# Splitting the first quarter of the next expert weights in two pieces, the first of them between a ReLU and a copy

## The chip, the cores and the metric

The kernel runs on one core of a Trainium2 chip. The metric is the device time of one execution in microseconds (us); lower is better. The engines are named as in the profile: PE (TensorE matmuls), PEld (its weight loads), ACT (ScalarE), DVE (VectorE), POOL (GpSimd), SP (SyncE, which issues transfers).

## The reference

Three stages: a thresholded attention, a dense layer with squared ReLU, and eight experts, of which each token takes one. The change touches the third:

```python
# N, D, E, F = 2304, 512, 8, 1024
logits = x @ w_gate
e_idx = np.argmax(logits, axis=1)
...
for e in range(E):
    mask = e_idx == e
    ...
    h = np.maximum(x[mask] @ w1[e], 0.0)
    ye = h @ w2[e]
    out[mask] = gate_w[mask, None] * eom[mask, e, None] * ye
```

Everything is in float32.

## The kernel before

A matmul in full float32 precision is replaced by three in a faster format (fp32r): each operand is split into a high part (a copy rounded to fp32r) and a low part (the operand minus its high part), and high x high, high x low and low x high are summed. So every operand is written twice before PE reads it: the high part by ACT, the low part by DVE or POOL.

The expert stage sorts the tokens by expert into *slots* of 128 tokens, each with one expert. There are at least 18 and at most 25 slots; how many there are, and which expert each has, is known only on the chip. With these inputs there are 22 (88 high-part copies of weights, four a slot). A slot's steps:

- the 128 rows of x are gathered (POOL's indirect DMA), transposed on PE into `xt_ps` and split into `x_gT_hi` (ACT) and `x_gT_lo` (DVE);
- `hidden`: two groups g = 0, 1 of 12 matmuls each (128x512) fill `he_ps0` and `he_ps1`;
- ACT applies the ReLU (`relu`, into `h_sb`), PE transposes four blocks for each group into `ht_ps`, ACT (`split_h`, into `h_T_hi`) and DVE (`h_T_lo`) split them;
- `output`: again two groups of 12 matmuls, into `oe_ps`; DVE scales the sum into `o_sb` and POOL stores it by indirect DMA.

The transposes stand inside the products: those of the first half of h after two of the four chunks of `hidden`'s second group, those of the second half after the first chunk of `output`. The next slot's x is transposed between `hidden` and `output`.

The weights of one expert are 128 x 8192 float32 in a raw buffer, of which there are three (`w_experts`). There is only one pair of split buffers, `w_hi` and `w_lo`, each in four quarters of 128 x 2048: quarters 0 and 1 are w1 (the two groups of `hidden`), 2 and 3 are w2 (the two groups of `output`). In every slot all four quarters are split anew for the next slot, each as soon as PE has finished with it. A quarter is written once the group that reads it is complete: semaphores `he_done` and `y_done` count these groups. ACT counts its high parts in `hi_done`, DVE its low parts (quarters 0 to 2) in `lo_dve`, POOL its (quarter 3) in `lo_pool`, and PE waits for `lo_dve` or `lo_pool` before each group.

The order of the work is written out by hand, one instruction stream for each engine. ACT's of a slot t (`slot` in the scalar block): high part of quarter 3 (of slot t's own weights), ReLU of the first half, copy of the first half of h, ReLU of the second half, copy of the next x, copy of the second half of h, and high parts of quarters 0, 1 and 2 for slot t + 1. DVE's: low part of the first half of h, of the next x, of the second half of h, low parts of quarters 0 and 1, the scaling, low part of quarter 2. The first slots and the last of the 18 sure ones are written out, the ones between run in a hardware loop (of three slots a pass on PE and DVE, one on ACT), and the slots behind the 18th stand in nested conditions. SP loads expert e + 3 into its buffer when POOL and DVE have split the last slot that uses expert e.

Of the kernel before, what the change touches and what calls it, by code (L numbers as in the profile page):

```python
# [19 lines left out]
ALU = mybir.AluOpType  # L20
# [935 lines left out]

RING = 3
BUF, NEED = 0, SLOTS
ENDS = 2 * SLOTS


def experts(nc, w1, w2, y_rows, out, con):
# [4 lines left out]
    with ExitStack() as ctx:  # L967
# [131 lines left out]

        def split_lo(eng, alu, t, g, buf, done):  # L1100
            eng.wait_ge(hi_done, 4 * t + g + 1)
            alu.tensor_tensor(group_of(w_lo, g), raw_group(buf, g), group_of(w_hi, g).bitcast(F32),  # L1102
                              ALU.subtract).then_inc(done, 1)

        @block.sync
        def _(sp):
# [4 lines left out]
            def load(e):  # L1111
                n = (e % BUFS) * WE
                if e >= BUFS:

                    end = sp.value_load(control[0:1, ENDS + e - BUFS:ENDS + e - BUFS + 1], min_val=0, max_val=SLOTS)
                    wait_first(sp, lo_dve, 3 * end + 1, sp_on)
                    wait_first(sp, lo_pool, end + 1, sp_on)
                sp.dma_start(w_raw[:, n:n + KC * FE].rearrange("p (c f) -> p c f", c=KC),
                             w1[e].rearrange("(c p) f -> p c f", p=P)).then_inc(w1_in[e % BUFS], 16)
                sp.dma_start(w_raw[:, n + KC * FE:n + WE].rearrange("p (c f) -> p c f", c=FEC),  # L1120
                             w2[e].rearrange("(c p) f -> p c f", p=P)).then_inc(w2_in[e % BUFS], 16)
# [22 lines left out]
        def _(pool):  # L1144
# [16 lines left out]
            def split(t):  # L1161
                buf = weight_buffer(pool, t)
                split_lo(pool, nc.gpsimd, t, 3, buf, lo_pool)

# [42 lines left out]
        def _(pe):  # L1207
# [26 lines left out]
            def products(out, lhs_hi, lhs_lo, c0, g, ahead_of=None, between=None):  # L1234

                for c in range(4):
                    if c == ahead_of:
                        between()
                    w = [x[:, g, c * 512:(c + 1) * 512] for x in (w_hi, w_lo)]
                    for n, (lhs, rhs) in enumerate(((lhs_hi, w[0]), (lhs_hi, w[1]), (lhs_lo, w[0]))):  # L1240
                        last = pe.matmul(out, lhs[:, c0 + c, :], rhs, start=(g != 3 and c == 0 and n == 0),  # L1241
                                         stop=(g != 2 and c == 3 and n == 2))
                return last

            def hidden(t):
# [3 lines left out]
                for g in range(2):  # L1249
                    pe.wait_ge(lo_dve, 3 * t + g + 2)  # L1250


                    products(h_ps[g][:], x_hi, x_lo, 0, g, ahead_of=2 if g else None,
                             between=lambda: h_transposed(t, 0)).then_inc(he_done, 1)
# [9 lines left out]
            def output(t, p):  # L1264
                pe.wait_ge(scaled, t + 1)
                for g in range(2):
                    pe.wait_ge(hlo_done, 2 * t + g + 1)
                    if g == 0:
                        pe.wait_ge(lo_dve, 3 * t + 4)
                    else:  # L1270
                        pe.wait_ge(lo_pool, t + 2)

                    products(oe_ps[p][:], h_hi, h_lo, 4 * g, 2 + g, ahead_of=None if g else 1,
                             between=lambda: h_transposed(t, 1)).then_inc(y_done, 1)
# [18 lines left out]
        def _(act):  # L1293
# [26 lines left out]

            def split_w(t, g, weights):
                buf, need = weights
                if g % 2 == 0:
                    wait_first(act, w1_ready if g == 0 else w2_ready, need, act_on)
                if not static(t) or t >= 1:

                    act.wait_ge(he_done if g < 2 else y_done, 2 * t - 1 + g % 2)  # L1327
                nc.scalar.activation(group_of(w_hi, g), raw_group(buf, g), ACT.Copy).then_inc(hi_done, 1)  # L1328

            def slot(t, first, more):  # L1330
                if not first:
                    split_w(t, 3, (weight_buffer(act, t), None))
                if more:
                    following = weights_of(t + 1)
                relu(t, 0)
                split_h(t, 0)
                relu(t, 1)
# [3 lines left out]
                if more:  # L1341
                    split_w(t + 1, 0, following)
                    split_w(t + 1, 1, following)
                    split_w(t + 1, 2, following)

            act.wait_ge(control_done, 1)
            weights = weights_of(0)
            split_w(0, 0, weights)
            split_w(0, 1, weights)
            split_x(0)  # L1350
            split_w(0, 2, weights)
            split_w(0, 3, weights)
            slot(0, True, True)
# [5 lines left out]
        def _(dve):  # L1359
# [101 lines left out]
            def slot(t, p, more):  # L1461
# [4 lines left out]
                if more:  # L1466
                    buf = weight_buffer(dve, t + 1)
                    split_lo(dve, nc.vector, t + 1, 0, buf, lo_dve)
                    split_lo(dve, nc.vector, t + 1, 1, buf, lo_dve)
                scale(t, p)  # L1470
                if more:
                    split_lo(dve, nc.vector, t + 1, 2, buf, lo_dve)

            buf = weight_buffer(dve, 0)
            split_lo(dve, nc.vector, 0, 0, buf, lo_dve)
            split_lo(dve, nc.vector, 0, 1, buf, lo_dve)
            split_x(0)
            split_lo(dve, nc.vector, 0, 2, buf, lo_dve)
            for t in range(RING):
# [41 lines left out]
```

## Time and profile before

| | us |
|---|---|
| median of 3 runs | 1074.66 (1074.55 to 1075.87) |
| profiled execution, its own time | 1075.23 |
| span of the profiled execution | 1073.4 |
| first matmul of the expert products to the last slot's first | 780.87 to 1052.14 |
| a slot, in the loop | 12.73 to 12.76 |
| PE busy over the span | 1017.6 (95%) |

Times of rows are us from the start of the span. A row of a timeline has the start, the duration, the engine, the line of the kernel, the operation, and output<-inputs. In brackets stands the idle time of the engine before it and what ended it. A matmul's row is longer than the interval to the next one, since matmuls are pipelined: the interval between starts is the time that one costs. PEld rows are the weight loads that run one matmul ahead.

### The profile page before, as it was taken

Reading aid. Unit: us, or ns where it says so; the run is one execution under the profiler, and the core shown is the slowest. Engines: PE = TensorE matmul, PEld = TensorE weight load, DVE = VectorE, ACT = ScalarE, POOL = GpSimd, SP = SyncE. Lnnn points to the kernel's source line nnn. Section 1 sums busy time; section 2 is a strip of 40 time slices with the busy share of each in tenths; the row PEclk is TensorE's granted clock in tenths of the full one; section 3 lists DMA queues with packets and bytes.
Section 4 is the critical chain, followed back from the end, with each engine's and each line's share of the span. In section 5 each row is a group of like instructions: output and inputs, shape, how many; then the busy total and the mean of one; then the engine's idle time right before and its main releaser. Section 6 shows DMA issues by size and latency. Waiting matters only on the chain. (4 is left out here: it accounts for less than half of the span.)

```text
span 1073.4 us, 19432 instructions
## 1 busy us (share of the span) xinstructions
PE 1017.6 (95%) x6901; PEld 840.3 (78%) x6901; DVE 612.5 (57%) x1137; ACT 596.3 (56%) x902; POOL 461.1 (43%) x725
## 2 busy tenths in 40 slices
PE   7999999999998999999999999999299999999996
PEld 5778778778776888888888888899177777777774
DVE  5788788888784334222422422332757777777773
ACT  4777787777774334222322322233168888877773
POOL 4777777777772000000000000000347777777773
PEclk9999999999999999999999999999589999999999
DMA  4322322323112110000000000010981554510110
GB/s 111 83 51 69 82 51 77 74 63 77 39 28 71 49 40 1 20 20 1 10 20 10 0 20 20 1 31 11 349 326 39 198 209 172 193 39 32 40 39 33
DMA packets 78891, 75.16 MB, mean 70 GB/s; under 512 B 49103, under 2 KB 59855, under 8 KB 78802
## 3 DMA queue, kind: packets, MB, share of 16 engines
q1 hardware_dynamic: 75282, 63.49, 19.7%
q0 software_dynamic: 3520, 10.49, 3.0%
q8 instruction: 54, 0.88, 0.4%
q14 instruction: 35, 0.29, 0.1%
HBM read 64.52 MB, written 10.49 MB: 70 GB/s over the span
## 5 line engine op out<-in xcount | busy, mean ns | idle before, releaser
L915 DVE TENSOR_TENSOR g_buf<-r_buf 128x512 f32<-128x512 f32 (+1 forms) x80 | 51.1, 639 | 236.1 <-ACT r_buf L853 236.1
L1165 POOL MEMSET ones<- 128x128 bf16 x1 | 0.2, 210 | 416.0 <-POOLq L652 416.0
L853 ACT ACTIVATE r_buf<-h_ps 128x512 f32<-128x512 f32 (+1 forms) x80 | 44.4, 556 | 240.0 <-PE h_ps L799 240.0
L1328 ACT ACTIVATE w_hi<-w_experts 128x2048 fp32r x88 | 161.1, 1906 | 13.2 <-issue 13.2
L1102 POOL TENSOR_TENSOR w_lo<-w_experts,w_hi 128x2048 fp32r<-128x2048 f32 x22 | 138.8, 6307 | 64.5 <-ACT w_hi L1328 64.5
L1102 DVE TENSOR_TENSOR w_lo<-w_experts,w_hi 128x2048 fp32r<-128x2048 f32 x66 | 149.1, 2286 | 28.0 <-ACT w_hi L1328 28.0
L478 ACT ACTIVATE e_sb<-s_sb,stats,live 128x576 f32<-128x576 f32 x144 | 124.5, 865 | 22.4 <-POOL stats L264 21.0
L799 PE MATMUL h_ps<-x_hi,w_in_hi 128*128 128x512 f32 (+1 forms) x320 | 120.2, 376 | 2.3 <-DVE x_lo L901 2.3
L799 PE MATMUL h_ps<-x_hi,w_in_lo 128*128 128x512 f32 (+1 forms) x320 | 118.6, 371 | 0.0
L799 PE MATMUL h_ps<-x_lo,w_in_hi 128*128 128x512 f32 (+1 forms) x320 | 118.5, 370 | 0.0
L816 PE MATMUL y_ps<-g_hi,w_out_hi 128*128 128x512 f32 (+1 forms) x320 | 117.9, 368 | 0.0
L816 PE MATMUL y_ps<-g_lo,w_out_hi 128*128 128x512 f32 (+1 forms) x320 | 117.7, 368 | 0.0
L816 PE MATMUL y_ps<-g_hi,w_out_lo 128*128 128x512 f32 (+1 forms) x320 | 117.7, 368 | 0.0
L577 DVE SCALAR_TENSOR_TENSOR probs<-s_sb,stats,e_sb 128x576 f32<-128x576 f32 x144 | 115.3, 833 | 1.5 <-POOL stats L277 1.4
L568 DVE TENSOR_SCALAR_CACHE_REDUCE s_sb<-s_ps 128x576 f32<-128x576 f32 x144 | 103.8, 754 | 19.8 <-PE s_ps L354 18.6
L496 ACT ACTIVATE probs_T<-t_ps 128x384 f32<-128x384 f32 x192 | 86.7, 486 | 33.3 <-PE t_ps L369 28.2
L264 POOL TENSOR_SCALAR stats<-stats,minus_live 128x1 f32<-128x1 f32 x144 | 76.4, 531 | 61.3 <-DVE s_sb L568 60.7
L369 PE MATMUL t_ps<-ident,probs 128*128 128x128 f32 x576 | 87.9, 280 | 6.7 <-ACT probs_T L496 6.6
L369 PEld LDWEIGHTS t_ps<-ident,probs 128*128 128x128 f32 x576 | 64.9, 142 | 18.3 <-issue 17.9
L1241 PE MATMUL he_ps<-w_hi,x_gT_hi 128*128 128x512 f32 x176 | 74.0, 420 | 5.2 <-DVE w_lo L1102 2.1
L1241 PE MATMUL oe_ps<-w_hi,h_T_hi 128*128 128x512 f32 x176 | 72.9, 414 | 0.1
L799 PEld LDWEIGHTS h_ps<-x_hi,w_in_hi 128*128 128x128 f32 x320 | 60.8, 190 | 12.4 <-ACT x_hi L838 2.4
(190 smaller groups left out, 2228.3 us busy)
## 6 DMA issues: line engine op xcount, KB each, us to landing
w_experts<-in_moe_w_dram SPq DMA_DIRECT2D x16, 2048.0 KB, 9.6
y_rows<-y_row SPq DMA_DIRECT2D x36, 128.0 KB, 2.4
k_raw<-in_k_dram SPq DMA_DIRECT2D x32, 128.0 KB, 3.1
q_raw<-in_q_dram SPq DMA_DIRECT2D x32, 128.0 KB, 2.9
w_raw<-in_moe_w_in_dram SPq DMA_DIRECT2D x16, 256.0 KB, 3.1
v_nat<-in_v_dram SPq DMA_DIRECT2D x16, 256.0 KB, 2.6
y_T<-in_moe_w_out_dram SPq DMA_DIRECT2D x16, 256.0 KB, 2.6
v_odd<-in_v_dram SPq DMA_DIRECT2D x16, 64.0 KB, 2.3
```

Source lines behind the costliest of these rows:

```text
L264: V.tensor_scalar(stat(BIAS, step, h), stat(MAX, step, h), minus_live[:], None, ALU.mult).then_inc(bias_ready, 1)
L369: last = pe.transpose(out[:, j * P:(j + 1) * P], probs[c][:, blk * P:(blk + 1) * P], ident[:])
L478: nc.scalar.activation(e_sb[step % 2][h][:], s_sb[step % 2][h][:], ACT.Exp, bias=stat(BIAS, step, h), scale=live[:]).then_inc(exp_done, 1)
L496: nc.scalar.activation(out, src[:], ACT.Copy).then_inc(evac_done, 1)
L568: V.tensor_scalar(halves(s_sb[step % 2][h][:]), s_ps[n % 2][:, :, 0:HALF], 1.0, None, ALU.mult, ALU.max, accum_out=stat(MAX, step, h)).the ...
L577: V.scalar_tensor_tensor(probs_of(c, h), s_sb[step % 2][h][:], stat(CUT, step, h), e_sb[step % 2][h][:], ALU.is_ge, ALU.mult, accum_out=su ...
L799: last = pe.matmul(h_ps[:, f % 2, 0:cols], w, x[:, kc, 0:cols], start=(kc == 0 and m == 0), stop=(kc == KC - 1 and m == 2))
L816: last = pe.matmul(y_ps[d][:, 0:cols], w, g[f % 2][:, 0:cols], start=(f == 0 and m == 0), stop=(f == FC - 1 and m == 2))
L915: V.tensor_tensor(g_buf[:, 0:cols], r_buf[:, 0:cols], r_buf[:, 0:cols], ALU.mult).then_inc(sq_done, 1)
L1102: alu.tensor_tensor(group_of(w_lo, g), raw_group(buf, g), group_of(w_hi, g).bitcast(F32), ALU.subtract).then_inc(done, 1)
L1241: last = pe.matmul(out, lhs[:, c0 + c, :], rhs, start=(g != 3 and c == 0 and n == 0), stop=(g != 2 and c == 3 and n == 2))
L1328: nc.scalar.activation(group_of(w_hi, g), raw_group(buf, g), ACT.Copy).then_inc(hi_done, 1)
```

## The change

The high and low part of quarter 0 are each made in two pieces of 128 x 1024 (the chunks 0 and 1, and 2 and 3). The first high piece goes between the ReLU and the copy of the first half of h on ACT, the second stays behind the copy of the second half of h, ahead of quarter 1. DVE makes both low pieces where the low part of quarter 0 was. A list `PARTS` numbers the five pieces (quarter, first chunk, end chunk), and the counts that PE, SP and the engines wait for are changed to it (4 low parts of DVE in each slot where there were 3, 5 high parts where there were 4). PE's own order does not change: `ahead_of` counts matmuls now and no chunks, at the same places.

```diff
+PARTS = ((0, 0, 2), (0, 2, 4), (1, 0, 4), (2, 0, 4), (3, 0, 4))
+NPARTS = len(PARTS)
...
-        def split_lo(eng, alu, t, g, buf, done):
-            eng.wait_ge(hi_done, 4 * t + g + 1)
-            alu.tensor_tensor(group_of(w_lo, g), raw_group(buf, g), group_of(w_hi, g).bitcast(F32),
-                              ALU.subtract).then_inc(done, 1)
+        def split_lo(eng, alu, t, part, buf, done):
+            g, c0, c1 = PARTS[part]
+            eng.wait_ge(hi_done, NPARTS * t + part + 1)
+            alu.tensor_tensor(group_of(w_lo, g)[:, c0:c1], raw_group(buf, g)[:, c0:c1],
+                              group_of(w_hi, g)[:, c0:c1].bitcast(F32), ALU.subtract).then_inc(done, 1)
...
-                    wait_first(sp, lo_dve, 3 * end + 1, sp_on)
+                    wait_first(sp, lo_dve, (NPARTS - 1) * end + 1, sp_on)
...
                 for c in range(4):
-                    if c == ahead_of:
-                        between()
                     w = [x[:, g, c * 512:(c + 1) * 512] for x in (w_hi, w_lo)]
                     for n, (lhs, rhs) in enumerate(((lhs_hi, w[0]), (lhs_hi, w[1]), (lhs_lo, w[0]))):
+                        if 3 * c + n == ahead_of:
+                            between()
...
                 for g in range(2):
-                    pe.wait_ge(lo_dve, 3 * t + g + 2)
-
-
-                    products(h_ps[g][:], x_hi, x_lo, 0, g, ahead_of=2 if g else None,
+                    pe.wait_ge(lo_dve, (NPARTS - 1) * t + g + 3)
+
+
+                    products(h_ps[g][:], x_hi, x_lo, 0, g, ahead_of=6 if g else None,
...
-            def split_w(t, g, weights):
+            def split_w(t, part, weights):
                 buf, need = weights
-                if g % 2 == 0:
+                g, c0, c1 = PARTS[part]
+                if c0 == 0 and g % 2 == 0:
                     wait_first(act, w1_ready if g == 0 else w2_ready, need, act_on)
                 if not static(t) or t >= 1:
 
                     act.wait_ge(he_done if g < 2 else y_done, 2 * t - 1 + g % 2)
-                nc.scalar.activation(group_of(w_hi, g), raw_group(buf, g), ACT.Copy).then_inc(hi_done, 1)
+                nc.scalar.activation(group_of(w_hi, g)[:, c0:c1], raw_group(buf, g)[:, c0:c1], ACT.Copy).then_inc(hi_done, 1)
 
             def slot(t, first, more):
                 if not first:
-                    split_w(t, 3, (weight_buffer(act, t), None))
+                    split_w(t, 4, (weight_buffer(act, t), None))
                 if more:
                     following = weights_of(t + 1)
                 relu(t, 0)
+                if more:
+                    split_w(t + 1, 0, following)
                 split_h(t, 0)
                 relu(t, 1)
                 if more:
                     split_x(t + 1)
                 split_h(t, 1)
                 if more:
-                    split_w(t + 1, 0, following)
                     split_w(t + 1, 1, following)
                     split_w(t + 1, 2, following)
+                    split_w(t + 1, 3, following)
...
                     split_lo(dve, nc.vector, t + 1, 0, buf, lo_dve)
                     split_lo(dve, nc.vector, t + 1, 1, buf, lo_dve)
+                    split_lo(dve, nc.vector, t + 1, 2, buf, lo_dve)
                 scale(t, p)
                 if more:
-                    split_lo(dve, nc.vector, t + 1, 2, buf, lo_dve)
+                    split_lo(dve, nc.vector, t + 1, 3, buf, lo_dve)
```

What ACT issues in one pass of its loop, from the first ReLU on, before the change (`h_sb` is the ReLU, `h_T_hi` the copy of h, ISA and REGISTER_ALU are address and counter instructions):

```order
L1309 ACTIVATE h_sb<-he_ps0 128x512 [waits ht_set]
L1315 ACTIVATE h_T_hi<-ht_ps0 128x512 [waits y_done,ht_set]
L1306 REGISTER_ALU
L1309 ACTIVATE h_sb<-he_ps1 128x512 [waits ht_set,he_done]
L1300 REGISTER_ALU
L1302 REGISTER_ALU [waits xt_set]
L1303 ACTIVATE x_gT_hi<-xt_ps 128x512 [waits he_done]
L1315 ACTIVATE h_T_hi<-ht_ps1 128x512 [waits y_done,ht_set]
L1327 REGISTER_ALU [waits w1_ready]
L1328 ISA [waits he_done]
L1328 ACTIVATE w_hi<-w_experts 128x2048
```

And in the changed kernel, where ACT's lines are 4 or 5 higher:

```order
L1313 ACTIVATE h_sb<-he_ps0 128x512 [waits ht_set]
L1332 ISA [waits w1_ready]
L1333 ISA [waits he_done]
L1333 ACTIVATE w_hi<-w_experts 128x1024
L1319 ACTIVATE h_T_hi<-ht_ps0 128x512 [waits y_done,ht_set]
L1310 REGISTER_ALU
L1313 ACTIVATE h_sb<-he_ps1 128x512 [waits ht_set,he_done]
L1304 REGISTER_ALU
L1307 ACTIVATE x_gT_hi<-xt_ps 128x512 [waits he_done,xt_set]
L1319 ACTIVATE h_T_hi<-ht_ps1 128x512 [waits y_done,ht_set]
L1333 ISA [waits he_done]
L1333 ACTIVATE w_hi<-w_experts 128x1024
```

One 128x1024 piece moved ahead of the copy of the first half of h, with its wait for the weights (`w1_ready`); the other stands where the whole quarter stood.

What DVE issues in one slot of its loop, before, from the low part of the second half of h on:

```order
L1447 TENSOR_TENSOR h_T_lo<-ht_ps1,h_T_hi 128x512 [waits h_T_hi_done]
L1074 TENSOR_LOAD control
L1074 ISA x2
L1102 ISA [waits hi_done]
L1102 TENSOR_TENSOR w_lo<-w_experts,w_hi 128x2048
L1102 ISA [waits hi_done]
L1102 TENSOR_TENSOR w_lo<-w_experts,w_hi 128x2048
L1458 TENSOR_SCALAR o_sb1<-oe_ps1,place_factor 128x512 [waits y_done]
L1102 ISA [waits hi_done]
L1102 TENSOR_TENSOR w_lo<-w_experts,w_hi 128x2048
```

And now:

```order
L1454 TENSOR_TENSOR h_T_lo<-ht_ps1,h_T_hi 128x512 [waits h_T_hi_done]
L1077 TENSOR_LOAD control
L1077 ISA x2
L1106 ISA [waits hi_done]
L1106 TENSOR_TENSOR w_lo<-w_experts,w_hi 128x1024
L1106 ISA [waits hi_done]
L1106 TENSOR_TENSOR w_lo<-w_experts,w_hi 128x1024
L1106 ISA [waits hi_done]
L1106 TENSOR_TENSOR w_lo<-w_experts,w_hi 128x2048
L1465 TENSOR_SCALAR o_sb1<-oe_ps1,place_factor 128x512 [waits y_done]
L1106 ISA [waits hi_done]
L1106 TENSOR_TENSOR w_lo<-w_experts,w_hi 128x2048
```

The first 128x2048 subtraction became two of 128x1024, one behind the other; nothing else moved on DVE.

## Rows read from the trace of the kernel before

**Rows 1.** The page: busy us, share of the span and instructions of each engine.

```profile
PE 1017.6 (95%) x6901; PEld 840.3 (78%) x6901; DVE 612.5 (57%) x1137; ACT 596.3 (56%) x902; POOL 461.1 (43%) x725
```

**Rows 2.** Windows: us; PE, PEld, DVE, ACT, POOL busy (instructions); clock, DMA, GB/s.

```profile
859.77:974.50 114.73, 113.77 (x540) 91.14 (x541) 84.86 (x64) 91.14 (x82) 90.16 (x28) 1.00 0.41 144
```

**Rows 3.** The chain of waits, in order of time: start us, us, what.

```profile
870.15 2.30 DVE w_lo L1102
...
974.50 4.38 PE he_ps L1241 x18
...
987.33 4.37 PE he_ps L1241 x18
...
1038.48 4.37 PE he_ps L1241 x18
```

**Rows 4.** Timeline at a slot boundary: start, us, engine, instruction [idle before <-releaser].

```profile
871.29 0.39 PE L1241 MATMUL oe_ps<-w_hi,h_T_lo 128*128 128x512 f32 x1
...
871.97 0.39 PE L1241 MATMUL oe_ps<-w_hi,h_T_lo 128*128 128x512 f32 x1
872.50 0.19 PEld L1241 LDWEIGHTS he_ps<-w_hi,x_gT_hi 128*128 128x128 f32 x1 [0.56 <-DVE w_lo L1102]
...
872.84 0.40 PE L1241 MATMUL he_ps<-w_lo,x_gT_hi 128*128 128x512 f32 x1
```

**Rows 5.** Waits of the weight loads, 790 to 1053: us, times, longest.

```profile
PEld he_ps L1241 <- DVE w_lo L1102: 8.0, 15, 0.6
PEld he_ps L1241 <- issue: 4.5, 6, 1.5
```

**Rows 6.** Timeline at a slot boundary behind the loop.

```profile
1012.32 0.39 PE L1241 MATMUL oe_ps<-w_hi,h_T_lo 128*128 128x512 f32 x1
...
1013.25 0.40 PE L1241 MATMUL he_ps<-w_lo,x_gT_hi 128*128 128x512 f32 x1
```

**Rows 7.** Timeline at the start of the last slot.

```profile
1052.11 0.19 PEld L1241 LDWEIGHTS he_ps<-w_hi,x_gT_hi 128*128 128x128 f32 x1 [1.45 <-issue]
```

**Rows 8.** Timeline of ACT through one slot.

```profile
862.89 0.60 ACT L1309 ACTIVATE h_sb<-he_ps 128x512 f32<-128x512 f32 x1 [0.21 <-PE he_ps L1241]
864.62 0.60 ACT L1315 ACTIVATE h_T_hi<-ht_ps 128x512 fp32r<-128x512 f32 x1 [1.12 <-PE ht_ps L1261]
866.02 0.60 ACT L1309 ACTIVATE h_sb<-he_ps 128x512 f32<-128x512 f32 x1 [0.80 <-PE he_ps L1241]
866.54 0.60 ACT L1303 ACTIVATE x_gT_hi<-xt_ps 128x512 fp32r<-128x512 f32 x1
...
868.10 7.31 ACT L1328 ACTIVATE w_hi<-w_experts 128x2048 fp32r x4
```

**Rows 9.** Timeline of PE at the start of the output product.

```profile
865.83 0.60 PE L1231 MATMUL xt_ps<-ident,x_g 128*128 128x128 f32 x4
...
866.18 0.19 PEld L1241 LDWEIGHTS oe_ps<-w_hi,h_T_hi 128*128 128x128 f32 x1
```

**Rows 10.** Timeline of DVE through the same slot.

```profile
865.25 0.69 DVE L1447 TENSOR_TENSOR h_T_lo<-ht_ps,h_T_hi 128x512 fp32r<-128x512 f32 x1 [0.48 <-ACT h_T_hi L1315]
...
868.24 0.69 DVE L1447 TENSOR_TENSOR h_T_lo<-ht_ps,h_T_hi 128x512 fp32r<-128x512 f32 x1 [0.38 <-ACT h_T_hi L1315]
870.15 4.49 DVE L1102 TENSOR_TENSOR w_lo<-w_experts,w_hi 128x2048 fp32r<-128x2048 f32 x2 [1.22 <-ACT w_hi L1328]
...
875.23 2.28 DVE L1102 TENSOR_TENSOR w_lo<-w_experts,w_hi 128x2048 fp32r<-128x2048 f32 x1
877.98 0.69 DVE L1447 TENSOR_TENSOR h_T_lo<-ht_ps,h_T_hi 128x512 fp32r<-128x512 f32 x1 [0.48 <-ACT h_T_hi L1315]
```

**Rows 11.** Timeline of POOL in the same slot.

```profile
862.89 6.38 POOL L1102 TENSOR_TENSOR w_lo<-w_experts,w_hi 128x2048 fp32r<-128x2048 f32 x1 [2.28 <-ACT w_hi L1328]
```

**Rows 12.** Weight load at the second half of the output product.

```profile
869.32 0.19 PEld L1241 LDWEIGHTS oe_ps<-w_hi,h_T_hi 128*128 128x128 f32 x1
```

**Rows 13.** The page: transfers of expert weights, KB each, us to landing.

```profile
w_experts<-in_moe_w_dram SPq DMA_DIRECT2D x16, 2048.0 KB, 9.6
```

More of the change, by code:

```diff
@@ L1162, in split @@
                 buf = weight_buffer(pool, t)
-                split_lo(pool, nc.gpsimd, t, 3, buf, lo_pool)
+                split_lo(pool, nc.gpsimd, t, NPARTS - 1, buf, lo_pool)
             nc.gpsimd.memset(ones[:], 1.0).then_inc(pool_set, 1)
@@ L1268, in output @@
                     if g == 0:
-                        pe.wait_ge(lo_dve, 3 * t + 4)
+                        pe.wait_ge(lo_dve, (NPARTS - 1) * (t + 1) + 1)
                     else:
                         pe.wait_ge(lo_pool, t + 2)
-                    products(oe_ps[p][:], h_hi, h_lo, 4 * g, 2 + g, ahead_of=None if g else 1,
+                    products(oe_ps[p][:], h_hi, h_lo, 4 * g, 2 + g, ahead_of=None if g else 3,
                              between=lambda: h_transposed(t, 1)).then_inc(y_done, 1)
@@ L1341, in slot @@
                 if more:
-                    split_w(t + 1, 0, following)
                     split_w(t + 1, 1, following)
                     split_w(t + 1, 2, following)
+                    split_w(t + 1, 3, following)
             act.wait_ge(control_done, 1)
             weights = weights_of(0)
-            split_w(0, 0, weights)
-            split_w(0, 1, weights)
+            for part in range(3):
+                split_w(0, part, weights)
             split_x(0)
-            split_w(0, 2, weights)
-            split_w(0, 3, weights)
+            for part in range(3, NPARTS):
+                split_w(0, part, weights)
             slot(0, True, True)
@@ L1469, in slot @@
                     split_lo(dve, nc.vector, t + 1, 1, buf, lo_dve)
+                    split_lo(dve, nc.vector, t + 1, 2, buf, lo_dve)
                 scale(t, p)
                 if more:
-                    split_lo(dve, nc.vector, t + 1, 2, buf, lo_dve)
+                    split_lo(dve, nc.vector, t + 1, 3, buf, lo_dve)
             buf = weight_buffer(dve, 0)
-            split_lo(dve, nc.vector, 0, 0, buf, lo_dve)
-            split_lo(dve, nc.vector, 0, 1, buf, lo_dve)
+            for part in range(3):
+                split_lo(dve, nc.vector, 0, part, buf, lo_dve)
             split_x(0)
-            split_lo(dve, nc.vector, 0, 2, buf, lo_dve)
+            split_lo(dve, nc.vector, 0, 3, buf, lo_dve)
             for t in range(RING):
```

## Prediction

> **What bounds the kernel now.** I read the page first. PE is busy for 95% of the span and the other engines for less than 60% [rows 1]; in nine slots of the expert stage it is busy 113.77 of 114.73 us, at a granted clock of 1.00, which is its 2.4 GHz level [rows 2]. So only what PE itself loses can be won, and it is small. Where it loses anything is told by the chain of waits [rows 3]: in each slot it leaves PE once, for a high part on ACT and a low part of 2.30 us on DVE that starts at 870.15 and ends at 872.45. This is the low part of quarter 0, which the first matmul of the next slot needs.
>
> The timeline shows the price. Near the end of a slot matmuls start every 0.227 us (871.29 to 871.97 is three of them) [rows 4]. Then the load of the next slot's first weights, which would have started with the matmul at 871.97, starts only at 872.50, 0.05 after the low part ended, and the second matmul of the slot starts at 872.84. From 871.97 to there are 0.87 us where two undisturbed intervals take 0.454: PE loses 0.42 us. It is two things, the wait (0.30) and a restart in which the first load is not hidden (0.11).
>
> The waits of the loads count such boundaries [rows 5]: 15 ended by DVE's low part, 8.0 us, and 6 ended by "issue", 4.5 us, of which the longest is 1.5. The 15 are those of the loop; they idle 0.533 us on average against 0.56 in the one I measured, so on average they lose 0.42 - 0.03 = 0.39 us. The other six lie behind the loop. Five of them are alike: from 1012.32 to 1013.25 are 0.93 us, so 0.93 - 0.454 = 0.48 lost, and (4.5 - 1.45) / 5 = 0.61 idle on average against about 0.62 here gives 0.465 each [rows 5, 6]. I read them as the same wait for DVE, with one more instruction of PE's queue behind it. The sixth, before the last slot, is 1.45 us long [rows 7] and starts 0.9 us after DVE is through; I read it as PE's branch to another place of the program, which no low part shortens.
>
> **The change, part by part.**
>
> *First high piece, now behind the first ReLU.* ACT idles 1.12 us between the ReLU at 862.89 and the copy of h at 864.62 [rows 8], because PE must transpose in between. The piece is let go by what releases the ReLU itself, the end of the first group of `hidden`. A back-to-back successor of a 128x512 operation starts 0.52 later (866.02 to 866.54), and one of 128x2048 occupies (7.31 - 1.91) / 3 = 1.80 [rows 8]. No row has 128x1024; its bounds are these two, and on the line between them it occupies 0.52 + 1.28 / 3 = 0.95, which I take. It then starts at 862.89 + 0.52 = 863.41 and frees ACT at 864.36, 0.26 before the copy of h can start. Cost nothing, and the cover is 0.26 us thick. At the lower bound the spare is 0.69; at the upper one the copy would be 0.59 late. What is queued behind it is just that copy, and this matters: DVE's low part of h ends at 865.25 + 0.69 = 865.94 [rows 10], PE's load for the output product follows at 866.18, 0.35 behind the start of the transposes of x [rows 9]. I cannot tell from the rows which of the two sets it, so I count no spare behind the copy of h: every 0.1 us of delay there is 0.1 us of PE.
>
> The Trainium skill, "VectorE: DVE Perf Modes", section "The TRN2 errata", speaks against just this edit: an operation that reads SBUF pays a fixed cost, exposed between instructions, so many small tiles pay it each. By its ScalarE formula, 224 cycles plus one for each element at 1.2 GHz, the piece would take 1.04 us, as an estimate, all of it after the ReLU's end at 863.49, and end at 864.53: the spare would shrink to 0.09 and the sum stay as it is. This case's rows show operations starting 0.08 us before their predecessor ends (866.54 against 866.62), so the measurement is milder than the page.
>
> *ACT after the second copy of h.* The four copies run from 868.10 to 875.41 [rows 8]. Now it is half a quarter and three: quarter 1 is done at 868.10 + 0.95 + 1.91 = 870.96, quarter 2 starts at 870.85, quarter 3 at 872.65 and ends at 874.56, 0.85 earlier than now. Quarter 3 must not start before the last matmul of the slot is through at 871.97 + 0.39 = 872.36 [rows 4]; it does not. ACT's total rises by the fixed part of one operation, 0.1 us, on an engine with time to spare.
>
> *DVE.* It is free at 868.24 + 0.69 = 868.93 and today idles until 870.15 for the high part [rows 10]. Both high pieces are done before (the second at about 869.15), so the first low piece can start once its address is read; between 868.93 and 870.15 I take 869.2. A subtraction of 2048 takes 2.28 and occupies 4.49 - 2.28 = 2.21; one of 512 takes 0.69 [rows 10]. These are the bounds for 1024; on the line it takes 1.22 and occupies 1.15. The second piece ends at 869.2 + 1.15 + 1.22 = 871.57, 0.88 earlier than 872.45 and 0.35 before 871.92, from which a load at 871.97 would be late. So the wait goes wholly, restart included. At the upper bound the pieces would end at 873.7 and make every slot longer; each would have to occupy over 1.3 before anything of the gain is lost, which neither neighbour suggests. Quarter 1's low part then ends at 873.8, the scaling at 874.5 and quarter 2's low part at 876.7, ahead of the next low part of h, today at 877.98 and 0.4 earlier then.
>
> *What is late next.* POOL's low part of quarter 3 runs 862.89 to 869.27 [rows 11], and PE's load that needs it starts at 869.32 [rows 12], 0.05 behind its end: this pair is at its edge today. A faster slot alone would run into it. But POOL starts 0.2 after ACT's quarter 3, which comes 0.85 earlier, while PE comes 0.4 earlier: POOL gains 0.45 us of spare. The Trainium skill, "GPSIMD Engine Reference", section "Key points", says that POOL shares its SBUF interfaces with DVE and contends with instructions of two SBUF inputs, which these subtractions are. The rows do not show it: a slot of (974.50 - 872.50) / 8 = 12.75 us later [rows 3, 4] POOL runs again, from 875.64 on, DVE's subtraction at 875.23 runs to 877.51 beside it and takes 2.28, and the two at 870.15, with no subtraction on POOL, take 4.49 together [rows 10, 11].
>
> *Weights.* ACT waits for the next expert's weights 4.7 us earlier (863.4 for 868.1). The transfers land in 9.6 us (median) [rows 13] and start when a buffer comes free, two experts, so at least two slots or 25 us, ahead of their use. Nothing.
>
> *Sum.* 15 x 0.39 = 5.85, and 5 x 0.465 = 2.3: 8.15 us. In the first slot PE waits for the gathered x, in the last for its branch: no change. The profiled execution took 1075.23, so 1067.1 as the profile would have it. The median of the runs is 0.57 lower than this execution; from it 1066.5, which I forecast. About 0.2% (2.1 us) is what a measurement of this kernel can tell from no change.
>
> **Rivals.**
>
> *A, the copy of h becomes late (slower).* If the piece occupies ACT as a whole quarter does, 1.80, it frees ACT at 865.21, the copy of h is 0.59 late in 20 slots, and PE stops before the output product, again with a restart of 0.1. The slot wins 0.41 and loses 0.69: 20 x 0.28 = 5.6 slower, 1080. It decides from an occupation of about 0.95 + 0.26 + 0.3 = 1.5. Against it: durations grow evenly with the elements in the two rows I have. For it: no row has this shape, and a wait for weights and an address instruction stand between ReLU and piece.
>
> *B, half of it.* The piece goes, but 0.1 to 0.25 us of delay reach PE in each slot, by the queue instructions ahead of the copy of h or by a fixed cost on either engine. 20 x 0.15 to 20 x 0.25 less: 3 to 5 us of gain, 1070 to 1071.5. For it is the missing spare behind the copy of h.
>
> *C, no change.* Something else is due at the same moment as the low part: the next x, or PE's branches at the loop's end and in the conditions, of which rows 7 show that one can cost 1.45. If DVE's address read keeps the first piece near its old start, 870.15, the second ends at 870.15 + 1.15 + 1.22 = 872.5, as now: 1074.7. Against it: DVE has idled long before 870.15 and its release there is the high part.
>
> *D, the five boundaries behind the loop are bound by PE's own issue*, as the row's label says, and give nothing: 15 x 0.39 = 5.85, so 1068.8.
>
> **How the numbers follow.** Full gain 0.6 (1065.5 to 1067.7), D 0.1, B 0.12, C 0.1, A 0.08. The likeliest is 1066.5. A range of 1065.0 to 1071.5 leaves out C and A, and takes in the full gain, D and most of B. Faster by over 0.2%: 0.6 + 0.1 + 0.12 less a little for the thin end of B, 0.8. Within 0.2%: 0.12. Slower: 0.08.
>
> **What would show it.** Right: the 15 waits of loads for DVE's low part are gone, the first load of a slot starts 0.227 after its neighbour, slots in the loop last 12.35; ACT's 128x1024 rows take about 1.03 and the copy of h still starts 0.1 or less behind PE's transposes; DVE's are about 1.22. Wrong: an idle of PEld before the output product, ended by DVE's low part of h (A, B), or one at the slot's start that ends with "issue" (C, D), or POOL's low part named as the one waited for.

## The result and the profile after

| | before | changed |
|---|---|---|
| median, same chip (6 runs each) | 1075.2 us | 1065.77 us |
| profiled execution, its own time | 1075.23 us | 1065.43 us |
| its span | 1073.4 us | 1063.7 us |
| a slot in the loop, mean of 15 (before / here) | 12.75 us | 12.32 us |
| a slot behind the loop, mean of 4 | 12.79 us | 12.28 us |

The ratio is 0.9912, with an interval of 0.9899 to 0.9925: 0.9% faster. The forecast was 1066.5 with a range of 1065.0 to 1071.5.

First the boundary between two slots in the timeline of the changed kernel, which answers to [rows 4]:

```profile
867.99 0.39 PE L1245 MATMUL oe_ps<-w_lo,h_T_hi 128*128 128x512 f32 x1
...
868.22 0.39 PE L1245 MATMUL oe_ps<-w_hi,h_T_lo 128*128 128x512 f32 x1
868.22 0.19 PEld L1245 LDWEIGHTS he_ps<-w_hi,x_gT_hi 128*128 128x128 f32 x1
868.44 0.39 PE L1245 MATMUL he_ps<-w_hi,x_gT_hi 128*128 128x512 f32 x1
...
868.67 0.39 PE L1245 MATMUL he_ps<-w_lo,x_gT_hi 128*128 128x512 f32 x1
```

The next slot's first load starts with the last matmul of the slot and has no bracket any more, which means that it does not wait; from 868.22 to 868.67 there are two plain intervals, where [rows 4] have 0.87 us. All waits of weight loads from 780 to 1053 us, answering to [rows 5]:

```profile
PEld he_ps L1245 <- DVE x_gT_lo L1459: 1.8, 1, 1.8
PEld he_ps L1245 <- issue: 1.5, 1, 1.5
PEld oe_ps L1245 <- issue: 0.5, 1, 0.5
```

The 15 waits for DVE's low part and five of the six "issue" waits are gone. What is left is the first slot's wait for its x and the one before the last slot; the 0.5 for `oe_ps` lies inside the last slot, which [rows 5] did not reach. The windows of nine loop slots and nearly five behind them show PE busy without a gap (busy us of PE first, then its loads, DVE, ACT and POOL, then the clock):

```profile
856.12:967.02 110.90, 110.90 (x541) 91.89 (x540) 85.48 (x73) 91.71 (x91) 75.65 (x27) 1.00 0.42 150
979.34:1040.00 60.66, 60.66 (x298) 50.35 (x297) 46.75 (x41) 50.21 (x51) 39.92 (x15) 1.00 0.12 40
```

Nine slots took 114.73 us before [rows 2] and take 110.90. The timeline of ACT through the slot from 856.12 on, answering to [rows 8]:

```profile
859.11 0.60 ACT L1313 ACTIVATE h_sb<-he_ps 128x512 f32<-128x512 f32 x1 [0.64 <-PE he_ps L1245]
859.61 1.05 ACT L1333 ACTIVATE w_hi<-w_experts 128x1024 fp32r x1
860.84 0.60 ACT L1319 ACTIVATE h_T_hi<-ht_ps 128x512 fp32r<-128x512 f32 x1 [0.18 <-PE ht_ps L1265]
...
864.32 6.47 ACT L1333 ACTIVATE w_hi<-w_experts 128x1024 fp32r x4
```

The last row holds the second piece and quarters 1 to 3 back to back: 6.47 us where the four whole quarters took 7.31, so quarter 3 is done 0.84 earlier (the prediction has 0.85). The first piece, 1.05 us long, fills the idle time between ReLU and copy and leaves 0.18 of it; the copy of h is still let go by PE's transposes, 1.73 us behind the ReLU's start as before (862.89 to 864.62 in [rows 8]). DVE in the same slot, answering to [rows 10]:

```profile
864.46 0.69 DVE L1454 TENSOR_TENSOR h_T_lo<-ht_ps,h_T_hi 128x512 fp32r<-128x512 f32 x1 [0.41 <-ACT h_T_hi L1319]
865.42 4.56 DVE L1106 TENSOR_TENSOR w_lo<-w_experts,w_hi 128x1024 fp32r<-128x1024 f32 x3 [0.27 <-ACT w_hi L1333]
```

The row of 4.56 us holds both low pieces and quarter 1's low part. It starts 0.27 after the low part of h, where DVE idled 1.22 before; each piece takes 1.22 (mean of 44). POOL, answering to [rows 11], and PE's load for the second output group, to [rows 12]:

```profile
858.68 6.30 POOL L1106 TENSOR_TENSOR w_lo<-w_experts,w_hi 128x2048 fp32r<-128x2048 f32 x1 [3.47 <-ACT w_hi L1333]
...
866.42 1.11 POOL L1161 DMA_INDIRECT out_dram<-o_sb,place_token  x1 [0.30 <-issue]
```

```profile
865.49 0.19 PEld L1245 LDWEIGHTS oe_ps<-w_hi,h_T_hi 128*128 128x128 f32 x1
```

POOL ends at 864.98, 0.51 ahead of the load that needs it; before it was 0.05. Its store took 1.11 us where it took about 2.6; I come back to that. Last, the idle time before the last slot, to [rows 7], and the same row of a second profile of the changed kernel:

```profile
1041.98 0.19 PEld L1245 LDWEIGHTS he_ps<-w_hi,x_gT_hi 128*128 128x128 f32 x1 [1.49 <-issue]
```

```profile
1041.19 0.19 PEld L1245 LDWEIGHTS he_ps<-w_hi,x_gT_hi 128*128 128x128 f32 x1 [0.84 <-issue]
```

The same program idles there 0.8 us in one execution and 1.5 in another. A compare-and-branch of PE's queue (0.08 us) ends 0.13 us before the load at 1041.98, so the branch does stand in this gap; what fills the 1.3 us ahead of it no row shows.

**Where 9.7 us of span went.** Slots 2 to 16 take 6.46 us less together (184.81 for 191.27), and slots 17 to 21 take 2.14 less (62.67 for 64.81). The boundary behind the first slot gave 0.4. These 9.0 us are the change. The other 0.7 are not: the first slot started 0.68 earlier after a program that is the same up to there, PE's granted clock rose from 0.5 (its 1.2 GHz level) to 1.0 after 9 matmuls of the first slot in place of 12 (0.45 us), and the end behind the last slot's start took 0.4 longer. In two more profiles of the changed kernel the first slot lasted 14.31 and 14.52 us (14.34 here), the end 21.3 both times (21.7 here), and a loop slot 12.31 and 12.32.

### The profile page after: what moved, and what is told of

It reads as the page before. It is cut to its first block and busy times, and to the rows that moved or that the text cites. A ratio compares the mean times of both kernels' runs of the same rounds, so it can differ in the third digit from the quotient of the medians.

```text
span 1063.7 us, 19532 instructions
## 1 busy us (share of the span) xinstructions
PE 1008.9 (95%) x6901; PEld 839.9 (79%) x6901; DVE 613.9 (58%) x1159; ACT 597.8 (56%) x924; POOL 428.6 (40%) x725
## 5 line engine op out<-in xcount | busy, mean ns | idle before, releaser
L1333 ACT ACTIVATE w_hi<-w_experts 128x2048 fp32r (+1 forms) x110 | 165.4, 1565 | 14.2 <-issue 14.2
L1106 POOL TENSOR_TENSOR w_lo<-w_experts,w_hi 128x2048 fp32r<-128x2048 f32 x22 | 134.8, 6128 | 86.4 <-ACT w_hi L1333 86.4
L1106 DVE TENSOR_TENSOR w_lo<-w_experts,w_hi 128x1024 fp32r<-128x1024 f32 (+1 forms) x88 | 150.6, 1753 | 5.9 <-ACT w_hi L1333 5.3
L1245 PE MATMUL he_ps<-w_hi,x_gT_hi 128*128 128x512 f32 x176 | 71.6, 407 | 2.5 <-DVE x_gT_lo L1459 1.4
L799 PEld LDWEIGHTS h_ps<-x_hi,w_in_hi 128*128 128x128 f32 x320 | 60.3, 189 | 12.3 <-ACT x_hi L838 2.4
```

The source lines that it names most:

```text
L799: last = pe.matmul(h_ps[:, f % 2, 0:cols], w, x[:, kc, 0:cols], start=(kc == 0 and m == 0), stop=(kc == KC - 1 and m == 2))
L1106: alu.tensor_tensor(group_of(w_lo, g)[:, c0:c1], raw_group(buf, g)[:, c0:c1], group_of(w_hi, g)[:, c0:c1].bitcast(F32), ALU.subtract).then ...
L1333: nc.scalar.activation(group_of(w_hi, g)[:, c0:c1], raw_group(buf, g)[:, c0:c1], ACT.Copy).then_inc(hi_done, 1)
```

## Experiments

My theory: the quarter's low part no longer arrives late because DVE need not wait for a whole high part; taking half of that high part out of ACT's row behind the second copy of h also brings quarter 3, and so POOL, forward in step with PE; and the piece just fits before a copy of h that has no time to give. Rivals: splitting alone, or moving alone, is enough, or the pieces on DVE matter. The move and the split are taken out one at a time below. All results together, slots as means over the profile, ratios against the kernel before on the same chip:

| kernel | median us | ratio, interval | loop slot | behind the loop |
|---|---|---|---|---|
| split, nothing moved | 1067.61 | 0.9930, 0.9914 to 0.9947 | 12.41 | 12.37 |
| the same, POOL half | 1065.30 | 0.9911, 0.9896 to 0.9926 | 12.32 | 12.28 |
| whole quarter moved | 1075.96 | 1.0011, 1.0002 to 1.0021 | 12.88 | 12.66 |
| low part whole | 1065.08 | 0.9908, 0.9892 to 0.9925 | 12.32 | 12.29 |
| pieces 3 and 1 | 1067.14 | 0.9928, 0.9912 to 0.9945 | 12.45 | 12.29 |
| pieces 1 and 3 | 1064.97 | 0.9908, 0.9893 to 0.9923 | 12.32 | 12.28 |
| changed, again | 1065.15 | 0.9915, 0.9901 to 0.9928 | 12.31 | 12.28 |
| changed, third time | 1065.00 | 0.9909, 0.9894 to 0.9924 | 12.32 | 12.28 |

**Split, nothing moved.**

```diff
                 relu(t, 0)
-                if more:
-                    split_w(t + 1, 0, following)
                 split_h(t, 0)
...
                 if more:
+                    split_w(t + 1, 0, following)
                     split_w(t + 1, 1, following)
```

> Quarter 0 is split in two pieces as in the changed kernel, but the first high piece stays behind the copy of the second half of h; nothing is moved ahead. My theory: the first piece would be ready at once for DVE, whose two low pieces end as early as in the changed kernel, so PE no longer waits for them. But ACT reaches quarter 3 0.9 us later, so POOL's low part of quarter 3 (6.3 us) ends about 22.2 us after the start of the slot before, where PE's load wants it at 21.7. Half of that difference stays in every slot, with a restart: slots in the loop of about 12.6 us, the load of the output product's second half ended by POOL's low part in the list of waits, and 1072 us in all, 2 to 4 us under the kernel before. Rival 1, splitting alone is enough: slots of 12.33 and about 1066. Rival 2, the early piece is needed for the low part of quarter 0: slots of 12.75, the load at the slot's start ended by DVE's low part, 1075.

Its median is 7.3 us under the kernel before, where the changed kernel's is 9.4 to 9.7 under it: more than I expected, and yet not all. The loop slot is 12.41 where I had said 12.6. No load waits for the low part of quarter 0, so rival 2 is out. Waits of loads in this kernel, without the two that every kernel has:

```profile
PEld oe_ps L1245 <- issue: 1.6, 6, 0.5
...
PEld oe_ps L1245 <- POOL w_lo L1106: 1.4, 8, 0.2
PEld xt_ps L1235 <- DMA x_g<-y_rows,place_token: 1.2, 2, 0.9
```

POOL's low part is late, as the theory says, by up to 0.2 and not by 0.5 (the waits that end with "issue" are the same load in the slots behind the loop, and one in the last slot). I had reckoned with 6.3 us for it; here it takes 5.97, and I had charged a restart that a load 0.2 late hardly costs. A gather of x that comes late is a second wait that I did not foresee, and it is half of the loss: over the 15 loop slots this kernel loses 1.29 us against the changed one, 0.65 of them in the one slot that waits 0.9 for its gather. The gather in question takes 1.91 us of POOL's time where the changed kernel's take 0.99, and the last section tells why:

```profile
842.98 1.91 POOL L1154 DMA_INDIRECT x_g<-y_rows,place_token  x1
```

**The same with half of POOL's work.**

```diff
+                if t == 0:
+                    split_lo(pool, nc.gpsimd, t, NPARTS - 1, buf, lo_pool)
+                    return
+                pool.wait_ge(hi_done, NPARTS * t + NPARTS)
+                nc.gpsimd.tensor_tensor(group_of(w_lo, 3)[:, 0:2], raw_group(buf, 3)[:, 0:2],
+                                        group_of(w_hi, 3)[:, 0:2].bitcast(F32), ALU.subtract).then_inc(lo_pool, 1)
```

> As the kernel with the split alone (nothing moved ahead), but from the second slot on POOL subtracts only half of quarter 3 (128x1024), and the other half of that low part keeps the values of the first slot. If POOL's low part is what holds the kernel with the split alone back, it is now 3 us early and slots in the loop last 12.33 us, about 1066 in all, as in the changed kernel. If that kernel is held back by the low part of quarter 0 or by ACT, nothing changes against it.

12.32 us and no wait left in the slots. This kernel leaves out half of a low part, and with it both the late subtraction and the late gather go, since POOL issues the gather behind the subtraction. So with the split alone POOL is the bound, by both, and the split alone frees PE of the low part of quarter 0. What the move adds is time for POOL (0.09 us a slot).

**The whole quarter moved, no split.** `PARTS` has its four quarters, one high and one low operation for each, and the waits count them.

> Quarter 0 is not split; its whole high part (128x2048) stands between the first ReLU and the copy of the first half of h. The low part of quarter 0 and POOL's are then as early as in the changed kernel, so the waits at the slot's start go. My theory says that there is no spare behind the copy of h: the high part frees ACT 0.58 us after the copy could start, so the output product starts 0.55 to 0.6 late with a restart of 0.1, slots in the loop of about 13.0 us, with a wait of PE's load of the output product for DVE's low part of h, 1079 to 1081 us in all. Rival, half a us of delay is hidden behind the transposes and matmuls of PE: slots of 12.33 to 12.5, about 1066 to 1069, and the split was not needed at all.

No gain at all: 1.0 us slower than before by the medians, at the edge of what these runs can tell, and under the 1079 to 1081 that I expected. PE and ACT around the output product's start:

```profile
863.95 1.91 ACT L1333 ACTIVATE w_hi<-w_experts 128x2048 fp32r x1
...
865.75 0.59 ACT L1319 ACTIVATE h_T_hi<-ht_ps 128x512 fp32r<-128x512 f32 x1
...
866.38 0.60 PE L1235 MATMUL xt_ps<-ident,x_g 128*128 128x128 f32 x4
...
867.30 0.19 PEld L1245 LDWEIGHTS oe_ps<-w_hi,h_T_hi 128*128 128x128 f32 x1 [0.56 <-issue]
```

The copy of h has no bracket: it follows the high part at once, 2.30 us behind the ReLU's start in place of 1.73. The load for the output product is 0.56 late. The slot loses 0.57 against the copy and lasts 0.55 longer than in the changed kernel, so nothing behind the copy absorbs anything, but the restart of 0.1 that I charged is not there. Behind the loop the slot is only 0.37 longer: there is a spare of 0.2 there which I had not seen. It has two parts. This load starts 0.23 us behind the end of DVE's low part of h in the loop and 0.07 behind it in the later slots, and ACT's first ReLU starts 3.00 us into a slot in the loop and 2.92 in most of the later ones.

**Pieces of three chunks and one.**

```diff
-PARTS = ((0, 0, 2), (0, 2, 4), (1, 0, 4), (2, 0, 4), (3, 0, 4))
+PARTS = ((0, 0, 3), (0, 3, 4), (1, 0, 4), (2, 0, 4), (3, 0, 4))
```

> As the changed kernel, with quarter 0 split in pieces of 128x1536 and 128x512 in place of two of 128x1024, so the piece ahead of the copy of h is longer. On the line through the rows it occupies ACT for 1.37 us and frees it 0.15 us after the copy of h could start. My theory (no spare behind that copy): slots in the loop of 12.45 to 12.6 us, 1068.5 to 1071 in all, and a start of the copy that follows the end of the piece and no longer PE's transposes. Rival, some tenths of spare: slots of 12.33 and 1066.

The timeline of ACT:

```profile
860.29 0.60 ACT L1313 ACTIVATE h_sb<-he_ps 128x512 f32<-128x512 f32 x1 [0.77 <-PE he_ps L1245]
860.78 1.48 ACT L1333 ACTIVATE w_hi<-w_experts 128x1536 fp32r x1
862.16 0.59 ACT L1319 ACTIVATE h_T_hi<-ht_ps 128x512 fp32r<-128x512 f32 x1
```

The copy starts 1.87 behind the ReLU's start, 0.14 late, and a loop slot is 0.13 longer. Behind the loop nothing is lost, by the spare just named. So 1067.1, under my range of 1068.5 to 1071, which took all slots alike and a restart.

**Pieces of one chunk and three.** The same edit with `(0, 0, 1), (0, 1, 4)`.

> As the changed kernel, with pieces of 128x512 and 128x1536. The early piece is shorter, so ACT comes to quarter 3 about 0.43 us later than in the changed kernel, and POOL's low part ends just when PE's load wants it (spare of 0.45 less 0.43). My theory: slots of 12.33 to 12.38, 1066 to 1067. If POOL had more spare than I count, 12.33 exactly; if the early piece matters by more than POOL (the low part of quarter 0 ends later), over 12.4. The early piece occupies ACT for 0.52 us.

The loop slot of 12.32 is at the lower end of what I expected, the whole 1.0 us under my 1066 to 1067. I had left POOL nothing to spare; it ended 0.4 us ahead of its load (860.55 + 5.96 = 866.51 for 866.91), since its subtraction took 5.96 and not 6.3.

**Low part whole.**

```diff
             g, c0, c1 = PARTS[part]
+            c0 = 0
...
-                    split_lo(dve, nc.vector, t + 1, 0, buf, lo_dve)
                     split_lo(dve, nc.vector, t + 1, 1, buf, lo_dve)
```

The counts for `lo_dve` are those of three low parts a slot again.

> As the changed kernel on ACT, but DVE makes the low part of quarter 0 in one operation of 128x2048, once both high pieces are there. My theory: the second high piece is ready when DVE comes to it anyway, so the one operation ends at the time of the two, which PE does not wait for: slots of 12.33 and the time of the changed kernel within 0.1%, about 1066. Rival, the two low pieces bring part of the gain: slots of 12.4 to 12.75. On the side: POOL's indirect store took 2.64 us in the kernel before and 1.11 in the changed one. If it waits for the end of the DVE subtraction that runs when it starts (in the kernel before 1.74 us to that end plus 0.9; in the changed one 0.22 plus 0.9), it takes about 2.2 us here; if it depends on something else, it stays near 1.1 or returns to 2.6.

With the first high piece moved ahead, the two pieces on DVE bring nothing: one operation does as well, because the second high piece is done by 865.37 (864.32 + 1.05), 0.2 after DVE comes free. Without the move both high pieces would end at about 866.3 in the changed kernel's times, and one whole subtraction at about 868.7, 0.4 behind the load at 868.22: an estimate from these rows. A kernel with the high part split, the low part whole and nothing moved was not run. The side question is answered too, in the last section.

**The changed kernel again.**

> The changed kernel once more, for a second profile and a comparison on one chip with the other runs. Between the two profiles in hand the spans differ by 9.7 us; I account 9.0 of it to slot boundaries (8.6 to 9.0 by theory again here) and the rest to execution-to-execution differences before the first slot (0.7) and to when the clock rises in the first slot (0.4), against a tail 0.4 longer. If that is so, the start of the first slot and the moment of the clock's rise move between profiles of one kernel, and the slots in the loop stay at 12.33.

> The changed kernel, for a comparison on the same chip with the three orders of transposes: 12.33 us a slot in the loop, 1065 to 1066 in all. Only the time before the first slot, the clock's rise in it and the branch before the last slot should differ from the profiles in hand.

Both as expected; the numbers stand above.

**A better version?** What PE still loses is the restart behind its three groups of transposes. I put two groups together:

```diff
+            def h_then_x(t, p, more):
+                h_transposed(t, 0)
+                if more:
+                    x_transposed(t + 1, (p + 1) % RING)
...
-                    products(h_ps[g][:], x_hi, x_lo, 0, g, ahead_of=6 if g else None,
-                             between=lambda: h_transposed(t, 0)).then_inc(he_done, 1)
+                    products(h_ps[g][:], x_hi, x_lo, 0, g, ahead_of=5 if g else None,
+                             between=lambda: h_then_x(t, p, more)).then_inc(he_done, 1)
```

> The changed kernel with another order on PE: the transposes of the next x stand directly behind those of the first half of h, and both one matmul earlier. In the changed kernel PE stops nowhere at slot boundaries; each of the three groups of transposes costs 0.36 us and a longer first matmul behind it (0.32 where 0.227 is usual), so putting two together can save 0.09 us for each slot. But the output product starts 0.24 us behind the low part of h, which is PE's own delay from release to load, so it can only start earlier if the transposes of h do. They may be 0.1 us earlier before they meet the end of the ReLU. Theory: slots of 12.23 to 12.3, 0.5 to 2 us less than the changed kernel. Rival: the ReLU's end holds the transposes and nothing is won or 0.1 us for each slot is lost.

1070.36 us (0.9956, 0.9942 to 0.9969), loop slots of 12.50 where I had hoped for 12.23 to 12.3, slower than the changed kernel. The transposes of x had stood between the second ReLU and the transposes of its result; without them these came too early:

```profile
PEld ht_ps L1270 <- ACT h_sb L1315: 9.0, 21, 0.4
```

Three more, with `output`'s transposes moved as well (the first number is the place in `hidden`, the second the one in `output`):

> The changed kernel with the transposes of the next x directly behind those of the first half of h, both one matmul earlier (after 5 of 12 of the second group of hidden), and the transposes of the second half of h after 5 matmuls of the output product in place of 3. The run with 5 and 3 lost 0.15 us a slot because those transposes then met the end of the second ReLU (PE's load waited 9.0 us in 21 slots for it). With 5 they stand as long behind the ReLU as in the changed kernel. Theory: no wait, one restart of 0.09 less a slot, slots of 12.23 to 12.26, 1.5 to 2 us less than the changed kernel. Rival: the low part of the second half of h, 0.1 us of spare before the second output group by my count, becomes late: slots of 12.3 to 12.35, no gain.

> As the run with 5 and 5, with the transposes of the second half of h after 4 matmuls of the output product. They come 0.92 us behind the end of hidden, the ReLU needs 0.65 and PE about 0.2 from its release to the load, so they just do not wait, and the low part of the second half of h has 0.2 us more spare than with 5. Theory: slots of 12.23 to 12.26, the best of the three. Rival: up to 0.1 us of wait at the ReLU, slots of 12.3 to 12.35.

> As 5 and 4, with the transposes of h and x after 6 matmuls of the second group of hidden, where those of h stand in the changed kernel. The output product would start 0.1 us earlier against the low part of h, behind which there is no spare. Theory: the saved restart comes back as a wait for the low part of h, slots of 12.30 to 12.36. Rival: the transposes of x ahead of the remaining matmuls leave the low part enough time, slots of 12.23 to 12.26.

| order | median us | ratio, interval | loop slot |
|---|---|---|---|
| 5 and 5 | 1068.52 | 0.9937, 0.9924 to 0.9951 | 12.52 |
| 5 and 4 | 1066.32 | 0.9918, 0.9904 to 0.9931 | 12.38 |
| 6 and 4 | 1066.57 | 0.9922, 0.9908 to 0.9935 | 12.41 |

With 5 and 5 the low part of the second half of h is late (rival), and most slots take 12.4 and more, above the rival's 12.3 to 12.35. With 5 and 4 six of the 15 loop slots last the 12.25 to 12.28 that I expected (behind the loop 12.27 on average), six take 12.30 to 12.33, and three 12.57, 12.59 and 13.05, so that the mean is above the changed kernel's. With 6 and 4 the slots are above my 12.30 to 12.36 too. In the waits of 5 and 4 the transposes of x stand with 1.4 us for a late gather, those of h with 0.2 us a slot:

```profile
PEld ht_ps L1270 <- ACT h_sb L1315: 4.3, 21, 0.2
...
PEld xt_ps L1235 <- DMA x_g<-y_rows,place_token: 1.4, 3, 0.8
```

The three long slots are the three that wait for a gather. Each of these gathers is issued within 0.5 us of a transfer of expert weights, the one that costs most here:

```profile
841.66 0.99 POOL L1154 DMA_INDIRECT x_g<-y_rows,place_token  x1 [0.16 <-issue]
```

```profile
841.59 0.37 SPq L1122 DMA_DIRECT2D w_experts<-in_moe_w_dram  x1
```

This gather lands 8.0 us after its start, at 849.69, and PE's load that waits for it starts at 849.73. In the changed kernel too the four gathers of the loop that are issued beside such a transfer take 6.9 to 8.1 us to land, all others of the loop 3.3 to 4.1; there the wait does not show, because the transposes of x come later in the slot. None of these orders beats the changed kernel.

## Why the prediction was right

- *The wait at the slot's start and its restart go*: right, in 20 boundaries of 20. The term was 8.15 us and the profile shows 9.0 (15 x 0.43 + 5 x 0.51). Each boundary was mis-sized by 0.04. I took the intervals behind the restart as plain, but the next six are longer too, 0.233 falling to 0.229 where 0.227 is usual, 0.03 in all (872.84, 873.07, 873.30, 873.53); in the changed kernel the first intervals are 0.227 at once. Another 0.02 lies in intervals near the end of the output product, 0.231 before and 0.227 now, whose cause stays open.
- *The number*: the forecast of 1066.5 lies 0.7 over the median of 1065.77, and part of that closeness is luck. It started from a median of three runs, 1074.66; from the 1075.2 of six runs the same sum gives 1067.05, 1.3 too high.
- *The five boundaries behind the loop are the same wait* (against rival D): right, though the row calls them "issue".
- *The last slot*: no gain by the change, but its wait is not a constant: 0.8 to 1.5 us over all the profiles.
- *The piece on ACT*: taken as 0.95 of occupation with 0.26 to spare. An operation queued behind a piece of this size does start 0.95 later (864.32 to 865.27), but the copy waits for PE, and what counts there is the piece's end: 1.05 long, 0.18 left idle. The Trainium skill, "VectorE: DVE Perf Modes", section "The TRN2 errata", gives 1.04 us by its ScalarE formula, and the trace agrees with 1.05 (mean of 44). The 0.09 to spare that I had added from it was too little, since the piece starts 0.10 before the ReLU's end.
- *No spare behind the copy of h*: shown for the loop by two runs (0.14 late costs 0.13, 0.57 costs 0.55). Wrong behind it, where 0.2 are to spare.
- *Rival A, a piece that occupies 1.80*: it was built, and costs 0.55 a loop slot, not 0.69, since no restart came on top. I had priced it at 1080; it is 1076, 1 us over the kernel before.
- *DVE*: 1.22 and 1.15 as interpolated; the low part ended 0.44 before the load (868.22 less 867.78); the prediction's 871.57 is 0.40 before 871.97. With the move, making two of it was without effect.
- *POOL gains 0.45*: 0.46 in the profile (0.51 to spare for 0.05). The sum took POOL's subtraction as a constant, and it is not; that it held is luck, since the time for which DVE's runs beside it hardly changed (1.9 and 1.83). That this is what the move is for, beside the split, I named as the next bound, and the run with the split alone bears it out; I had made the ACT piece and DVE's start the heart of it, and there the split alone does most: 7.3 of 9.4 us.
- *DVE and POOL don't contend*: wrong. The rows that I used give only DVE's durations, in a case where DVE's subtraction began first (875.23, and POOL's 0.4 later); POOL is the one that loses, see the last section. It did not change the sum, since POOL had time.

## What to carry to other kernels

A chain of two engines that each handle a whole tile costs the first engine's full operation before the second can begin: halve both, and the second starts half an operation earlier. Halving the first alone was enough here only because its first half had also been moved ahead. Before making one wait go, ask which other was just met (here POOL, 0.05 us ahead of its load) and whether the same edit moves it too. Work fits into an engine's idle gap only up to the gap: here 0.14 us over cost 0.13 in every loop slot, and a whole tile in place of half ate the entire gain.

## What the runs showed of the hardware

**POOL's store waits for DVE's subtraction.** The store to `out_dram` took about 2.64 us before and 1.11 after, and I wondered why. Before, it was

```profile
870.71 2.63 POOL L1157 DMA_INDIRECT out_dram<-o_sb,place_token  x1 [0.30 <-issue]
```

The run with the low part whole decides it. DVE's subtraction in that kernel, and POOL's store beside it:

```profile
867.04 2.29 DVE L1107 TENSOR_TENSOR w_lo<-w_experts,w_hi 128x2048 fp32r<-128x2048 f32 x1 [0.36 <-ACT w_hi L1334]
```

```profile
867.99 2.24 POOL L1162 DMA_INDIRECT out_dram<-o_sb,place_token  x1 [0.30 <-issue]
```

The subtraction ends at 869.33, 1.34 behind the store's start, and 2.24 less 1.34 is 0.90. In the kernel before the store began at 870.71, DVE's first subtraction ended at 872.45, and 1.74 + 0.9 is 2.64; in the changed one the piece that ran at 866.42 ended at 866.64, and 0.22 + 0.9 is 1.12. The stores in the kernel with three chunks and one (the subtraction ended 0.89 after the start, 1.79 in all) fit as well. A store that meets no subtraction takes 1.0, and so does one that starts before the subtraction does: with the split alone DVE's begins 0.36 after the store, which takes 1.02. The gathers follow the same rule. With the split alone most of them start 0.1 to 0.2 us behind DVE's first piece, which ends 1.0 to 1.1 after their start, and they take 1.9 us.

**POOL's subtraction stands still meanwhile.** Over all the profiles its duration for 128x2048 is 4.45 us plus the time for which one of DVE's weight subtractions runs beside it, within 0.05: 6.38 with 1.9 us of overlap before, 6.30 in the changed kernel with 1.83, 5.97 with 1.5 in the one with the split alone, and in the changed kernel's last slot, where only 0.6 overlap:

```profile
1044.36 5.07 POOL L1106 TENSOR_TENSOR w_lo<-w_experts,w_hi 128x2048 fp32r<-128x2048 f32 x1 [6.04 <-ACT w_hi L1333]
```

DVE's subtractions of weights do not lengthen (2.28 to 2.29 in every kernel). But in each of these overlaps of 0.4 us and more it is DVE's subtraction that began first, in the changed kernel's slot 0.45 us ahead of POOL's at 858.68:

```profile
858.23 2.28 DVE L1106 TENSOR_TENSOR w_lo<-w_experts,w_hi 128x2048 fp32r<-128x2048 f32 x1
```

So the rows show that POOL's stands still until the one that DVE had begun is through. Which side loses when POOL's begins first, no run shows. DVE's subtractions of h and x read one operand from PSUM and add nothing to POOL's time in the fit (they take 0.69 as ever); they also begin after POOL's, so that these runs cannot tell which of the two reasons it is. I missed the contention because I looked at DVE's durations alone. The Trainium skill, "GPSIMD Engine Reference", section "Key points", has the contention: POOL shares its SBUF interfaces with DVE and contends with DVE instructions of two SBUF inputs. I had dismissed the rule on rows that could not show POOL's side; this case's trace agrees with it, by 1.83 us of POOL's 6.30 in a slot of the changed kernel.
